# Zeroing only the unused result tiles of a routed layer after the routing is known, and splitting two weight blocks two experts earlier

## The reference

```python
# 1: attention, 4 batches x 8 heads x 576 positions x 64, causal by blocks of 64
scores = where(block_i >= block_j, q @ k.T / 8, -1e9)
attn = exp(scores - max);  attn /= attn.sum() + 1e-9
x = (attn @ v) as rows [2304, 512]
# 2: routed layer, 8 experts (512 -> 1024 -> 512)
do_compute = x @ w_skip > 0          # a token that is not computed keeps its x
e = argmax(x @ w_gate);  g = softmax(x @ w_gate)[e]
out = x + g * (relu(x @ w1[e]) @ w2[e])
# 3: dense layer, 512 -> 2048 -> 512
h = out @ w_in;  h = max(h, 0) + alpha * min(h, 0);  result = h @ w_out
```

## Time and profile before

| | |
|---|---|
| median of three runs | 871.87 us |
| the profiled execution | 871.87 us |
| its span | 870.0 us |
| TensorE busy | 817.1 us (94%) |
| TensorE weight load busy | 721.9 us (83%) |
| VectorE, ScalarE, GpSimd busy | 446.4, 274.5, 190.4 us |
| mean granted TensorE clock | 0.976 |
| bytes moved by DMA | 95.76 MB |

### The profile page before, as it was taken

One profiled execution on the slowest core, in us unless ns is written; L12 is line 12 of the kernel. 1 busy time (PEld: TensorE's weight loads), 2 busy tenths in 40 slices (PEclk: granted clock), 3 DMA queues, 4 the chain that ended last, 5 costly groups with the idle time before them and its releaser, 6 DMA issues.

```text
span 870.0 us, 15697 instructions
## 1 busy us (share of the span) xinstructions
PE 817.1 (94%) x5281; PEld 721.9 (83%) x5282; DVE 446.4 (51%) x916; ACT 274.5 (32%) x650; POOL 190.4 (22%) x191
## 2 busy tenths in 40 slices
PE   5999999999749999999769999999999999999997
PEld 4788888888549989989659889989998998998996
DVE  3777777777874444226544734543544434444432
ACT  5666665666333333133311121111112112112111
POOL 6242424422011143014178810000001001000000
PEclk9999999999959999999969999999999999999999
DMA  6678888675417766149433110002002002000001
GB/s 140 160 188 222 215 229 234 164 208 166 141 39 242 273 234 227 50 169 323 148 108 99 60 44 29 0 2 70 0 0 72 0 0 72 0 0 36 1 1 37
DMA packets 94599, 95.76 MB, mean 110 GB/s; under 512 B 64112, under 2 KB 65264, under 8 KB 94064
## 3 DMA queue, kind: packets, MB, share of 16 engines
q1 hardware_dynamic: 86000, 67.65, 27.4%
q0 software_dynamic: 4208, 14.95, 5.8%
q10 hardware_dynamic: 4368, 12.88, 4.0%
HBM read 64.78 MB, written 20.19 MB: 98 GB/s over the span
## 4 chain that ended last, share of the span: by engine, by line
PE 86%; DVE 4%; DMA 3%; ACT 3%; issue 2%; POOL 0%; SPq 0%; ACTq 0%; DVEq 0%; POOLq 0%
PE bank L920 23%; PE bank L931 22%; PE bank L870 9%; PE bank L884 8%; PE bank L751 6%; PE bank L762 4%; PE bank L739 3%; PE bank L715 2%; PE bank L733 2%; PE bank L786 2%; DMA w_sb<-in_moe_w_dram 1%; ACT p_sb L976 1%; PE bank L768 1%; PE bank L908 1%; PE bank L857 1%
## 5 line engine op out<-in xcount | busy, mean ns | idle before, releaser
L1412 DVE TENSOR_SCALAR g_sb<-bank,alpha_sb 128x384 f32<-128x384 f32 x96 | 59.3, 618 | 218.7 <-PE bank L920 218.6
L1088 ACT CAST g_hi<-g_sb 128x384 fp32r<-128x384 f32 x96 | 49.5, 515 | 321.8 <-DVE g_sb L1414 321.8
L920 PE MATMUL bank<-u_hi,wi_hi 128*128 128x384 f32 x384 | 130.5, 340 | 1.4 <-DVE u_lo L1385 1.4
L920 PE MATMUL bank<-u_hi,wi_lo 128*128 128x384 f32 x384 | 130.4, 340 | 0.0
L920 PE MATMUL bank<-u_lo,wi_hi 128*128 128x384 f32 x384 | 130.0, 339 | 0.0
L931 PE MATMUL bank<-wo_lo,g_hi 128*128 128x512 f32 x288 | 113.7, 395 | 0.0
L931 PE MATMUL bank<-wo_hi,g_lo 128*128 128x512 f32 x288 | 113.5, 394 | 0.0
L931 PE MATMUL bank<-wo_hi,g_hi 128*128 128x512 f32 x288 | 112.7, 391 | 0.8 <-DVE g_lo L1418 0.8
L870 PEld LDWEIGHTS bank<-rows_t,w_sb 128*128 128x128 f32 x832 | 97.6, 197 | 2.6 <-DVE rows_t L1329 1.5
L870 PE MATMUL bank<-rows_t,w_sb 128*128 128x128 f32 x832 | 97.9, 280 | 1.1 <-DVE rows_t L1329 1.1
L976 ACT ACTIVATE p_sb<-bank,neg_max 128x128 f32<-128x128 f32 (+2 forms) x144 | 79.1, 551 | 48.6 <-DVE neg_max L1117 46.1
(11 more groups left out here) (171 smaller groups left out, 1230.2 us busy)
## 6 DMA issues: line engine op xcount, KB each, us to landing
w_sb<-in_moe_w_dram ACTq DMA_DIRECT2D x6, 2048.0 KB, 8.0
w_sb<-in_moe_w_dram SPq DMA_DIRECT2D x6, 2048.0 KB, 10.8
q_t<-q_t SPq DMA_DIRECT2D x64, 160.0 KB, 2.5
w_sb<-in_moe_w_dram SPq DMA_DIRECT2D x16, 512.0 KB, 4.8
v_nat<-in_v_dram SPq DMA_DIRECT2D x32, 128.0 KB, 2.4
y_out<-in_moe_w_out_dram POOLq DMA_DIRECT2D x16, 256.0 KB, 3.0
out_dram<-y_out SPq DMA_DIRECT2D x16, 256.0 KB, 2.8
qk_nat<-in_q_dram SPq DMA_DIRECT2D x30, 128.0 KB, 4.0
```

What stands on the lines that cost most here:

```text
L920: last = pe.matmul(dst, w[:, j, P * f:P * f + P], u[:, j, :], start=z == 0, stop=z == len(terms) - 1)
L1088: act.copy(g_hi[:, f % GB, :], g_sb[:, f % 2, :]).then_inc(g_hi_done, 1)
L1412: dve.tensor_scalar(g, a, 0.0, alpha_sb[:, f:f + 1], ALU.min, ALU.mult).then_inc(neg_done, 1)
```

## The change

No tile is zeroed during attention. Once `routed` is signalled, SyncE reads `tile_hi[7]` from SBUF, waits until the rows of the first tile have been gathered (`rows_loaded` at 16), and then zeroes the unused tiles one by one in a loop, ahead of the loop that stores results. GpSimd waits for exactly as many of these DMAs before the gathers from `y_slots`; VectorE computes that number, 28 less the tiles in use, with one more instruction. Separately, GpSimd's two blocks of w_in are loaded and split at experts 1 and 3 in place of 3 and 5.

```diff
+        tile_free = sb("tile_free", [1, 1], I32)
...
-        REST_TILES = 3
-        LAST_TILES = SLOT_TILES - 2 * KD - REST_TILES * (PAIRS - 3 - 2 * KD)
...
-            def zero_tiles(at, count):
-
-                if count == 1:
-                    dst, src = y_slots[bass.ds(at * P, P), :], zeros[:]
-                else:
-                    dst = y_slots.rearrange("(t p) d -> p t d", p=P)[:, bass.ds(at, count), :]
-                    src = zeros[:].unsqueeze(1).to_broadcast([P, count, D])
-                sp.dma_start(dst, src).then_inc(y_zeroed, 16)
...
                     load_step(m + KD * par)
-                    zero_tiles(m + KD * par - 1, 1)
...
                 load_step(n)
-                zero_tiles(2 * KD + (n - 2 * KD - 1) * REST_TILES, REST_TILES)
                 save_tile(n - KD - 1)
             load_step(PAIRS - 2)
-            zero_tiles(SLOT_TILES - LAST_TILES, LAST_TILES)
...
             sp.wait_ge(routed, 1)
-            sp.wait_ge(y_zeroed, 16 * (PAIRS - 2))
+            used = sp.value_load(tile_hi[0:1, E - 1:E], min_val=1, max_val=MAX_TILES)
+            sp.wait_ge(rows_loaded, 16)
+            with sp.Fori(used, SLOT_TILES) as g:
+                sp.dma_start(y_slots[bass.ds(g * P, P), :], zeros[:]).then_inc(y_zeroed, 16)
...
             for e in range(E):
-                t, odd = divmod(e - 2, 2)
-                if odd and 0 <= t < LATE:
+                t, odd = divmod(e, 2)
+                if odd and t < LATE:
                     if t:
                         pool.wait_ge(wi_split, t)
                     pool.dma_start(stage[:, 0, :], wi_v[t]).then_inc(wi_loaded, 16)
                 tiles(e)
-                if odd and 0 <= t < LATE:
+                if odd and t < LATE:
                     pool.wait_ge(second_split, e + 1)
                     wi_rows(t)
...
             pool.wait_ge(back_ready, 1)
+            unused = pool.value_load(tile_free[0:1, 0:1], min_val=2, max_val=SLOT_TILES - 1)
+            pool.wait_ge(y_zeroed, 16 * unused)
             pool.wait_ge(rows_loaded, 16 * last + 32)
...
             step(dve.tensor_tensor(gate[:], total[:], active[:], ALU.mult))

+            dve.tensor_scalar(tile_free[:], hi_f[0:1, E - 1:E], -1.0, float(SLOT_TILES), ALU.mult, ALU.add)
             step(dve.tensor_scalar(from_f[:], slot_f[:], -float(SKIPPED), None, ALU.add))
```

## The result

The kernel after takes 881.63 us (median of 4 runs, 879.44 to 882.66) against 871.83 us (4 runs, 871.43 to 872.79): a ratio of 1.0108, 95% interval [1.0086, 1.0130]. It is slower by 9.8 us, where 872.2 us and no change had been forecast, and the time lies above the range of 871.3 to 874.2 us. The profiled execution took 883.74 us, its span is 881.7 us.

What follows compares the result with a forecast made beforehand. TensorE, busy 94% of the span, was taken to bound the kernel; span 870.0 plus 0.3 for expert 2's w2, all else 0, plus 1.87 around it, gave 872.2 us, no change; range 871.3 to 874.2.

Steps and rivals of the forecast that it cites:

- weights of expert 2 come really late: Rival at expert 2's first w2 matmul: w2 lands late, price up to 4.4 us, typical time 874.5 us; 14%.
- Attention gained nothing: Zeroing taken out of attention: TensorE waits for no DMA there, gain taken as 0, at most 0.6 us.
- VectorE's extra instruction: Between the gate and from_f: later tiles' numbers come 0.08 us later; cost 0, bound 0 to 0.1 us.
- the 264.7 that decides: Second gather: cost 0 if landed by 264.7; rival, held behind all zero writes, costs 2.3 us, 874.2; 4%.
- The split on GpSimd: Rival at expert 1: split gets in VectorE's way; if the block lands late, 0.9 us, 872.8 us; 10%.
- At the end GpSimd idles: Before the first gather from y_slots: register load and wait for zeros fit in 9.59 us of idle time; cost 0.
- writing goes on from about 254.5 to 266 or 267: Fifteen zero DMAs in the new place: 3.93 MB at 363 GB/s take 10.8 us; cost 0.
- the slow loop: SyncE's zero loop: issues 0.81 us apart, last at 264.4; at 1.0 us each, last at 267.
- the delay is up to twice as long: 1.0 to 2.0 us: w2 of expert 2 behind the early w_in block: delay less 1.4 us slack, stall 0 to 0.6, taken 0.3 us.
- the share between queues as even in bytes: w2 of expert 2 beside w1 of expert 3: even sharing doubles the delay, stall 0.6 rather than 0.3 us.
- The upper end, 4.4 us: Expert 2's w2 stall if nothing of 272 to 278 us is usable and sharing is even: 2 x 2.9 - 1.4.
- waits for rows named under "wrong": Sign against the forecast: TensorE waiting over 1 us for rows or h_lo between 265 and 305 us.

Runs made afterwards that it cites:

- seven_late: Kernel after, but the last eight tiles zeroed during attention by one DMA, seven left for the loop; 872.55 us, ratio 1.0004.
- early_start: Kernel after without SyncE's wait for the first gather in front of the zero loop; 873.48 us, ratio 1.0014.
- block_only: Kernel before with the w_in blocks loaded and split at experts 1 and 3, all zeroing still in attention; 872.99 us against 872.26, 1.0013.
- zero_only: Kernel after with the w_in blocks back at experts 3 and 5, zeroing still in the new place; 874.55 us against 872.26, 1.0024.
- w1_wait: Kernel after, but ScalarE issues w1 of expert 3 only when w2 of expert 2 has landed; 876.04 us against 871.88, 1.0035.
- eleven_late: Kernel after, but four unused tiles zeroed during attention by one early DMA, eleven left for the loop; 877.61 us against 872.93, 1.0052.
- eleven_wait: eleven_late, with ScalarE issuing w1 of expert 3 only once w2 of expert 2 has landed; 873.23 us against 872.92, 1.0004.
- before_again: The kernel before, unchanged, run and profiled once more; 872.06 us.
- zero_last: Kernel after, but the fifteen zero DMAs issued behind the last expert's w2; 874.46 us against 872.92, 1.0012.
- w1_halves: Kernel after with each later w1 load issued as two halves of its columns, rows of 2 KB instead of 4 KB; 880.46 us, 1.0091.
- zeros_pool: Kernel after with the zero loop on GpSimd's queue, ahead of its loop over the experts, instead of SyncE's; 881.60 us, 1.0114.
- stage_parts: Kernel after with the w_in block loaded in four parts, rows a quarter as long; 881.33 us against 872.93, 1.0095.

## Why the prediction was wrong

**Right.** The place and the mechanism of the loss were named, as the rival "weights of expert 2 come really late", with 14% and a price up to 4.4 us. Attention gained nothing by losing its zeroing. VectorE's extra instruction has its neighbour 0.08 us behind it. The rows of the second tile were copied at 263.12, before the 264.7 that decides. The split on GpSimd (278.53 to 286.80) lay between VectorE's two operations with two SBUF inputs, the one up to 278.44 and the one at 295.49, so that rival was not put to the test. At the end GpSimd idles 10.35 us before the first gather from y_slots, 9.59 before:
```profile
444.74 1.02 POOL L651 DMA_INDIRECT u_sb<-y_slots,from_i  x1 [10.35 <-POOLq L643]
```

**The step that failed first: "writing goes on from about 254.5 to 266 or 267".** It went on to 280.9. Two terms were off. The start was at 255.55, and the fourteen steps from first to last issue took 15.13 us, 1.08 each, above even the 1.0 that I had set as the slow loop. So the last zeros were issued at 270.7, not 264.4: a loop whose bound and address come from registers is not priced by two different DMAs of one loop body. And I divided the sum of the bytes by the full rate, as if the zeros had the engines alone until they were done. From 268 the w_in block and from 271 w1 of expert 2 were there and took 77% (268 to 271 us) and 70% (272 to 276 us) of the bytes of the two queues. seven_late and early_start, whose zeros are out at 264, show both terms harmless if the loop ends before these loads.

**The step that failed most: "the delay is up to twice as long: 1.0 to 2.0 us".** It was 8.0 us (18.3 against 10.3). The sum held only the block's bytes, with the zeros at nothing, since they were to be out at 267. That was the wrong way round: the block alone delays the landing by 0.1 us (block_only), the zeros alone by 3.8 (zero_only), both by 8.0. With both and w1 of expert 3 held back it is 3.6 (w1_wait), so 3.6 us come from the zeros and loads ahead and 4.4 from the w1 beside. And in that sharing too a size was off. I took the share between queues as even in bytes. The Trainium skill (page "DMA: Bandwidth & Descriptors", section "Queues, rings and completion order") says that an engine goes round its queues by packets; I read "even" from it. The trace speaks against my reading: the counts are nearly even (448 and 388 at 284 to 290 us), the bytes are 1 to 1.7 there and 1 to 3.4 beside the block. That fits turns of equal numbers of these packets; the page's packet holds several descriptors, and no run here shows how many packets of the trace make one turn. w1_wait shows what the neighbour costs: without it, and with all the zeros, 5.6 of 9.8 us go.

**What I had not seen: it is a cliff.** w1 of expert 3 is issued behind ScalarE's last evacuation of expert 1, so at a time that TensorE sets, and comes on 3.6 us later (280.58 and 284.2). A w2 that is nearly through by then on every engine doesn't notice (before, block_only, early_start, seven_late: 10.1 to 10.7 us). One that is not takes 2.7 times as long for the remainder (153 GB/s and not 410). Hence the interaction of two parts that are cheap alone. The spread of eleven_late's runs would follow too, if they stand on the edge; only one of them was traced, so this is not shown. In the kernel after the bulk of w2 is late on all engines (the 8th increment at 16.4 us, the last at 18.3). In zero_only and eleven_late half of the engines are through at 10.0 and 9.6 us, and it is the engine furthest behind that decides, not the bytes in sum. Why a few engines fall behind stays open: the records don't say which engine a packet was on.

**A term left out: the clock.** The upper end, 4.4 us, held only the stall. TensorE stopped at 293.45 and next worked at 297.83; in between, at 295.8, its granted clock fell to 0.50, and the 24 matmuls took 8.41 instead of 5.60 us. Where the group came 0.8 us late (eleven_wait) and 2.2 (zero_only) the clock stayed at 1.00 and it took 5.86 and 5.87 us; where it came 2.75 us late (w1_wait) the clock did fall and it took 7.42. So the 9.3 us are 5.8 us of idle time (4.38 + 1.43) and 3.5 of slower work: 2.8 in the group, 0.5 in the transposes ahead of it (1.12 us and not 0.60), the rest in small gaps. The waits for rows named under "wrong" came too, though not by a slow gather: ScalarE's copy stood behind the rounding of the late w2.

**The profiled execution's 11.87 us** over that of before are more than the 9.8 of the medians. 1.62 us stand already at the first w2 group (267.52 and 265.90); with 6.49 + 2.81 it is 10.9 behind expert 2's group, 10.5 at the first gather from y_slots (444.74 and 434.25), and 11.7 at the end of the span. The 1.62 us come from the start of the program, where the full clock is granted at a varying time: by the trace's first clock records at 12.0 us before and at 19.3 in the kernel after, where the first pair of matmuls takes 0.66 us and not 0.41. The first row of the chain stands between 25.79 and 28.21 us in the thirteen kernels (the two, and the eleven changed ones above) and at 27.09 in before_again, which is the same program as before. No step of the change hangs on it.

## What to carry to other kernels

When bulk writes are moved beside a weight stream, don't add bytes and divide by the rate. For each stretch list the queues that have work, take equal packet counts for them as these traces had, so that short rows lose to long ones, and ask what the squeezed load meets if it isn't done when the next one starts. Look at the last of a load's sixteen increments, not at their mean. Put such writes where a stretch ends without a deadline behind it (attention, or behind the last weights, as zero_last, whose 1.5 us are not clear of nothing), or let the next load wait for the one that is needed first (eleven_wait). Price a stall of several us with the slow clock after it, and follow what else stands behind the late load in each engine's queue: here the copy of rows.

## What the runs showed of the hardware that I had not expected

- Two queues with work on the same DMA engines had nearly equal numbers of packets, whatever their size: 401 and 399 with both at 2 KB (w1_halves), 272 and 272 with 2 KB against 4 KB (286 to 290 us of the kernel after), 130 and 110 with 2 KB against 8 KB. In eleven_late, where only a few engines had work for one of the queues, it was 54 against 282.
- GpSimd's queue carries rows of 2 KB as packets of 4 KB (the gathers, the zeros of zeros_pool, the parts of stage_parts); SyncE's queue carries them as 2 KB.
- A load issued while the engines are busy sends its first packet later. For w1 of expert 2 it was 1.1 us after the issue in the kernel before (265.80 and 266.90, DMA share 0.03 from 264 to 267) and 3.7 us in the kernel after (267.42 and 271.15, share 0.92 from 267 to 270).
- A loop on SyncE with bounds and addresses from registers issued a DMA each 1.08 us in the kernel after (15.13 / 14), 1.02 in early_start (14.35 / 14) and 0.92 in zero_last (12.86 / 14).
- The last of a load's sixteen increments can come several us behind the others: 3.3 us behind the fifteenth in zero_only, 4.0 in eleven_late (7.6 behind the eighth).
